# Delta-rule attention with two expert stages: attention's loop written out and its slot reordered

## The reference, cut to what matters

```python
# attention: 4 x 8 heads, 768 steps, head size 48
for t in range(S):
    y[:, :, t] = einsum('bhd,bhde->bhe', q[:, :, t], state)
    v_old = einsum('bhde,bhd->bhe', state, k_n[:, :, t])
    state += beta[t] * einsum('bhd,bhe->bhde', k_n[:, :, t], v[:, :, t] - v_old)
x = y as (3072 tokens, 384)
out = sum_e p_e * (relu(x @ w1[e]) @ w2[e])        # 4 experts, 384 -> 1024 -> 384
out = (sigmoid(out @ w_gate) * (out @ w_val)) @ w_out   # 384 -> 1536 -> 384
```

## Time and profile before

| | us |
|---|---|
| three timed runs | 1962.07, 1930.34, 1958.16 |
| their median | 1958.16 |
| the profiled execution | 1943.01 |
| its span, first to last instruction | 1940.7 |
| attention, from the start to the end of slot 11 and the tail | about 664 |
| slots 1 to 10, ten slots | 517.9 |

### The profile page before, as it was taken

The page is one execution under the profiler, slowest core; times in us unless marked ns, Lnnn a source line. Parts: engine busy times, 40 slices in busy tenths (PEclk is TensorE's granted clock), DMA queues, the critical chain, the costliest instruction groups (busy, mean ns, idle before and its releaser), DMA issues. The chain is left out here.

```text
span 1940.7 us, 42069 instructions
## 1 busy us (share of the span) xinstructions
PE 1838.7 (95%) x18050; PEld 1579.6 (81%) x18050; DVE 662.0 (34%) x1269; ACT 497.8 (26%) x944; POOL 66.4 (3%) x51
## 2 busy tenths in 40 slices
PE   5899989898999799999999999999998999999999
PEld 4677767676677689999999999999997888888888
DVE  6555545454554222222222222222224422222221
ACT  2443334333332121112111121111113322222222
POOL 1000000000000103000300030000000000000000
PEclk9887768787777699999999999999999999999999
DMA  7222222222000321022110301020102100000000
GB/s 154 46 55 48 52 54 54 54 54 54 18 19 19 115 98 66 33 71 91 49 50 32 130 33 66 33 89 33 66 0 73 49 17 17 1 16 16 0 17 17
DMA packets 145512, 95.11 MB, mean 49 GB/s; under 512 B 80944, under 2 KB 125232, under 8 KB 145360
## 3 DMA queue, kind: packets, MB, share of 16 engines
q1 hardware_dynamic: 145360, 92.77, 16.9%
HBM read 78.59 MB, written 14.16 MB: 48 GB/s over the span
## 5 line engine op out<-in xcount | busy, mean ns | idle before, releaser
L947 DVE SCALAR_TENSOR_TENSOR hl<-ebank,hh 128x512 fp32r<-128x512 f32 x192 | 132.9, 692 | 577.0 <-ACT hh L904 577.0
L904 ACT ACTIVATE hh<-ebank 128x512 fp32r<-128x512 f32 x192 | 115.0, 599 | 664.7 <-PE ebank L976 664.7
L974 PE MATMUL ebank<-w2l,hh 128*128 128x384 f32 x768 | 258.6, 337 | 4.1 <-DVE w2l L925 2.3
L976 PE MATMUL ebank<-w2h,hh 128*128 128x384 f32 x768 | 258.6, 337 | 0.0
L975 PE MATMUL ebank<-w2h,hl 128*128 128x384 f32 x768 | 257.8, 336 | 0.0
L974 PE MATMUL ebank<-xl,w1h 128*128 128x512 f32 x576 | 224.7, 390 | 12.2 <-DMA xl<-x_lo 12.2
L976 PE MATMUL ebank<-xh,w1h 128*128 128x512 f32 x576 | 228.0, 396 | 0.0
L975 PE MATMUL ebank<-xh,w1l 128*128 128x512 f32 x576 | 227.6, 395 | 0.0
L605 PE MATMUL bank<-c 128*128 128x256 f16 x576 | 141.7, 318 | 46.5 <-ACT XX L379 22.4
L974 PEld LDWEIGHTS ebank<-w2l,hh 128*128 128x128 f32 x768 | 144.3, 188 | 12.5 <-DVE w2l L925 2.8
L975 PEld LDWEIGHTS ebank<-w2h,hl 128*128 128x128 f32 x768 | 144.2, 188 | 7.0
(11 more groups left out here) (144 smaller groups left out, 2718.4 us busy)
## 6 DMA issues: line engine op xcount, KB each, us to landing
xh<-x_hi SPq DMA_DIRECT2D x24, 768.0 KB, 4.4
xl<-x_lo SPq DMA_DIRECT2D x24, 768.0 KB, 6.0
brep<-in_beta SPq DMA_DIRECT2D x24, 256.0 KB, 5.1
w1raw<-in_moe_w SPq DMA_DIRECT2D x4, 1536.0 KB, 9.6
w2raw<-in_moe_w SPq DMA_DIRECT2D x4, 1536.0 KB, 12.0
k_raw<-in_k SPq DMA_DIRECT2D x12, 384.0 KB, 4.7
v_raw<-in_v SPq DMA_DIRECT2D x12, 384.0 KB, 6.0
q<-in_q SPq DMA_DIRECT2D x12, 384.0 KB, 4.4
```

The costliest lines, as they stand in the source:

```text
L904: nc.scalar.activation(hs[i][0][:, :], bank[i][:, :], ACT.Relu).then_inc(hh_done, 1)
L947: nc.vector.scalar_tensor_tensor(out=hs[i][1][:, :], in0=bank[i][:, :], scalar=0.0, in1=hs[i][0][:, :].bitcast(F32), op0=ALU.max, op1=ALU. ...
L974: mm(dst, stat[0], mov[1], start=first, stop=False)
L976: return mm(dst, stat[0], mov[0], start=False, stop=last)
```

## The change

The loop is gone: all twelve slots are written out, on all engines. In the slot:

- on PE, dense pieces and tile steps are dealt out anew. `u0(0)` stands right behind `first(0)`; `turn(0)` and `turn(1)` move up, to right behind `z1(0)` and `z1(1)`; `s(1)` moves between `m32y(0)` and `m32y(1)`;
- `product_q` is split into its matmuls and, one step later, its mask on DVE (`mask_q`);
- `keep` moves from the slot before to the slot itself;
- the copies of the four quadrants into `XTf` leave `z3` and become a step of their own, `quads`, behind both `m32y`: ACT makes two of the four, DVE the other two;
- `Rf` is made by GpSimd;
- `busy` matmuls: one in place of two in `y1` to `y3`, `z0` to `z3`, `m32y` and `m64y`, none in `y0`. A slot has 28 of them.

```diff
             lev("first", w, p, 0)
+            r("u0", 0)
             lev("first", w, p, 1)
-            r("u0", 0)
+            pre("product_q", w, p, 0)
             lev("y0", w, p, 0)
+            pre("keep", w, p, None)
             n("square")
             r("u0", 1)
             lev("y0", w, p, 1)
-            pre("product_q", w, p, 0)
+            pre("mask_q", w, p, 0)
             lev("z0", w, p, 0)
...
             lev("z1", w, p, 0)
             n("unit", 0)
+            n("turn", 0)
             lev("z1", w, p, 1)
             n("unit", 1)
+            n("turn", 1)
             lev("y2", w, p, 0)
-            n("turn", 0)
+            r("u2", 0)
             lev("y2", w, p, 1)
-            r("u2", 0)
-            n("turn", 1)
+            n("product", 0)
...
             lev("m32y", w, p, 0)
+            r("s", 1)
             lev("m32y", w, p, 1)
-            r("s", 1)
-            n("keep")
+            lev("quads", w, p, 0)
             lev("m32z", w, p, 0)
             rec("z", w, p, 0)
+            lev("quads", w, p, 1)
             lev("m32z", w, p, 1)
             rec("z", w, p, 1)
             lev("m64y", w, p, 0)
             n("turn_q", 0)
             lev("m64y", w, p, 1)
+            lev("m64z", w, p, 0)
             n("turn_q", 1)
-            lev("m64z", w, p, 0)
             lev("m64z", w, p, 1)
...
-            slot(0, 0, lev, rec, pre, has_rec=False)
-            slot(1, 1, lev, rec, pre)
-            slot(2, 0, lev, rec, pre)
-            with eng.Fori(2, NCH) as c:
-                slot(2 * c - 1, 1, lev, rec, pre)
-                slot(2 * c, 0, lev, rec, pre)
-            slot(NW - 1, 1, lev, rec, pre, has_pre=False)
+            for w in range(NW):
+                slot(w, w % 2, lev, rec, pre, has_rec=w > 0, has_pre=w < NW - 1)
...
+                def rec(step, w, p, o):
+                    if step == "z":
+                        pool.wait_ge(r_done, 2 * w + o + 1)
+                        nc.gpsimd.tensor_copy(Rf[o][:, :, :], R[o][:, :, :]).then_inc(rf_done, 1)
...
-                    if step == "z3":
-                        if isinstance(w, int) and w < 2:
+                    if step == "quads":
+                        if w < 2:
                             act.wait_ge(x_zeroed, 1)
                         past(act, u2_rdy, 2 * (w - 1))
                         act.wait_ge(xt_done, 10 * w + 8 + hf + 1)
-                        for b in range(NB):
+                        for b in (2, 3):
...
+                    if step == "quads":
+                        past(dve, u2_rdy, 2 * (w - 1))
+                        for b in range(2):
+                            nc.vector.tensor_copy(XTf[p][quarter(b), half(hf), quarter(b)], XX[hf][quarter(b), 1, :, :])
...
                             pe.wait_ge(x1_done, 2 * w + hf + 1)
-                        busy(ybank[hf])
...
+                        pe.wait_ge(xt_done, 10 * w + 2 * n + hf + 1)
                         busy(xbank[hf])
-                        pe.wait_ge(xt_done, 10 * w + 2 * n + hf + 1)
                         pe.wait_ge(yc_done, 8 * w + 2 * n + hf + 1)
-                        busy(ybank[hf])
```

More of the change, by code:

```diff
@@ L206, in slot @@
             lev("y1", w, p, 1)
+            pre("mask_q", w, p, 1)
             r("au", 1)
@@ L219, in slot @@
             lev("z2", w, p, 1)
-            n("product", 0)
+            r("y", 0)
             lev("y3", w, p, 0)
-            r("y", 0)
+            n("product", 1)
             lev("y3", w, p, 1)
             n("value")
-            n("product", 1)
+            r("y", 1)
             lev("z3", w, p, 0)
-            r("y", 1)
             lev("z3", w, p, 1)
@@ L240, in slot, with run @@
             lev("m64y", w, p, 1)
+            lev("m64z", w, p, 0)
             n("turn_q", 1)
-            lev("m64z", w, p, 0)
             lev("m64z", w, p, 1)
-        def run(eng, lev, rec, pre):
+        def run(lev, rec, pre):
             for step, which in (("square", None), ("norm", None), ("value", None), ("unit", 0), ("unit", 1),
-                                ("turn", 0), ("turn", 1), ("product", 0), ("product", 1), ("keep", None),
+                                ("turn", 0), ("turn", 1), ("product", 0), ("product", 1),
                                 ("turn_q", 0), ("turn_q", 1)):
                 pre(step, 0, 0, which)
-            slot(0, 0, lev, rec, pre, has_rec=False)
-            slot(1, 1, lev, rec, pre)
-            slot(2, 0, lev, rec, pre)
-            with eng.Fori(2, NCH) as c:
-                slot(2 * c - 1, 1, lev, rec, pre)
-                slot(2 * c, 0, lev, rec, pre)
-            slot(NW - 1, 1, lev, rec, pre, has_pre=False)
+            for w in range(NW):
+                slot(w, w % 2, lev, rec, pre, has_rec=w > 0, has_pre=w < NW - 1)
             for step in ("u0", "au", "u2", "y"):
@@ L346, in _ @@
                 reload(0, 1, 0)
[L347 to L357, removed]
+                for w in range(1, NW):
+                    if w + 2 < NW:
+                        reload(w, w // 2 + 1, w % 2)
+                    for o in range(2):
+                        store(w - 1, (w - 1) // 2, (w - 1) % 2, o)
+                for o in range(2):
+                    store(NW - 1, NCH - 1, 1, o)
                 for o in range(2):
@@ L370, in _, with none @@
                 last.then_inc(s_zeroed, 1)
+                def rec(step, w, p, o):
+                    if step == "z":
+                        pool.wait_ge(r_done, 2 * w + o + 1)
+                        nc.gpsimd.tensor_copy(Rf[o][:, :, :], R[o][:, :, :]).then_inc(rf_done, 1)
+                def none(*_):
+                    return
+                run(none, rec, none)
             @block.scalar
@@ L410, in rec @@
                 def rec(step, w, p, o):
-                    if step == "z":
-                        act.wait_ge(r_done, 2 * w + o + 1)
-                        copy(Rf[o][:, :, :], R[o][:, :, :]).then_inc(rf_done, 1)
                     if step == "u0":
@@ L447, in pre @@
                         copy(Ah[p][:, half(which), :], A32[p][:, half(which), :], ASC).then_inc(ah_done, 1)
-                run(act, lev, rec, pre)
+                run(lev, rec, pre)
             @block.vector
@@ L510, in rec @@
                         past(dve, ds_rdy, 2 * (w - 1) + o + 1)
-                        if isinstance(w, int) and w == 0:
+                        if w == 0:
                             dve.wait_ge(s_zeroed, 1)
@@ L577, in pre @@
                                                     ALU.mult).then_inc(ap_done, 1)
-                    if step == "product_q":
+                    if step == "mask_q":
                         dve.wait_ge(qp_rdy, 2 * w + which + 1)
@@ L587, in _ @@
                 last.then_inc(x_zeroed, 1)
-                run(dve, lev, rec, pre)
+                run(lev, rec, pre)
             @block.tensor
@@ L610, in lev @@
                     if step == "first":
-                        if isinstance(w, int) and w == 0 and hf == 0:
+                        if w == 0 and hf == 0:
                             pe.wait_ge(consts_in, 32)
@@ L785, in pre @@
                         product(which, 1).then_inc(qp_rdy, 1)
-                run(pe, lev, rec, pre)
+                run(lev, rec, pre)
 def experts(nc, x_hi, x_lo, w1, w2, probs, acc, w1raw, w2raw, w1_in, ahead):
```

6 lines of the change are left out of this document (2 added, 4 removed).

## The result

The changed kernel takes **2001.86 us** (median of four runs, 1983.86 to 2009.36), the kernel before 1953.59 in the same comparison (four runs, 1930.34 to 1962.07): ratio 1.0274, 95% interval 1.0148 to 1.0401. It is slower; the interval leaves open whether by more or by less than 2%. The forecast was 1914 us, with a range up to 1980.

A forecast was written before the change was run, and what follows sets the result against it. PE was taken to bound the attention slots, by its clock, its waits for ACT and "issue" gaps. 1943.0 - 16.6 - 24 - 36.7 + 13 + 5.5 + 35 - 10 = 1909, plus 5: 1914 us, range 1868 to 1980.

The forecast's parts named there:

- Loop written out, -16.6: In attention, PE's three double "issue" gaps at the branches after slots 4, 6 and 8 go: -16.6 us.
- Busy matmuls, -24: Leaving out 20 of 48 busy matmuls a slot saves 0.10 to 0.11 us each at full clock: -24 us.
- Quadrants behind `Yc`, -36.7: PE's waits for ACT in m32y(1) and m32z(0) go entirely: -36.7 us.
- `z(0)`, +13: PE waits 1.1 to 1.2 us for S(0) from DVE ahead of z(0), in eleven slots: +13 us.
- `m64y(1)`, +5.5: DVE's quads copies delay m64y(1) by between nothing and 1.05 us; half taken: +5.5 us.
- `Rf` on GpSimd, 0: GpSimd's copy is hidden, as u0(0) reads it only some 4 us later: 0 us.
- the rival built on it: GpSimd locks DVE out in quads(1), 0.4 to 1.0 us ahead of m32z(1): 1922 us or so, chance 0.09.
- `turn` moved up, +35: PE waits for ku 1.5 us at turn(0) and 1.9 us at turn(1), in eleven slots: +35 us.
- Clock, -10: Half-clock time in slots 1 to 10 costs 6.9 us a slot against 8.3 before: -14, taken as -10 us.
- I take it back at the end of `y(0)`: The clock lost at the turns returns at the end of y(0), after 11 us at half, costing 4.3 us.
- Until it returns in m64 or in `product_q(0)` that is 8.5 us at half: The wait ahead of z(0) takes the clock in perhaps three slots of four, for 8.5 us, costing 2.6.
- the clock doesn't return: PE stays at 1.2 GHz from the turns to the next slot's product_q: +88 us, 2002 us, chance 0.14.

The follow-up runs named there:

- experiment 1: The kernel before with only its loop written out; 1921.5 us, ratio 0.9859.
- experiment 4: The kernel before with its loop written out and the quadrant copies moved behind Yc, shared by ACT and DVE, nothing else; 1904.7 us, ratio 0.9762.
- experiment 6: The kernel of experiment 4 with 28 busy matmuls a slot in place of 48, placed as in the change; 1916.5 us, ratio 0.9784.
- Experiment 2: The changed kernel with turn, u2, product and y back at their places of before; 1939.4 us, ratio 0.9956.
- 7: The kernel of experiment 4 with only the start of the slot spread as in the change, 48 busy matmuls; 1902.9 us, ratio 0.9747.
- (10): The changed kernel with twelve busy matmuls ahead of each turn's wait for ku, from slot 1 on; 1886.1 us, ratio 0.9614.
- experiment 9: The changed kernel with both unit steps moved earlier, right behind norm, turns left in place; 1878.9 us.
- experiment 11: The kernel of experiment 4 with XTf copied by GpSimd, XTb by ACT, and twelve more busy matmuls a slot; 1850.3 us, ratio 0.9482.
- experiment 3: The changed kernel with its 48 busy matmuls a slot put back; 2012.9 us.
- experiment 12: The changed kernel with both unit steps early, XTf on GpSimd, XTb on ACT and 48 busy matmuls a slot; 1817.6 us, ratio 0.9293.

## Why the prediction was wrong

*Loop written out, -16.6*: right, with a few us more by the clock; alone it gave 23 us by the medians (experiment 1). That written-out slots show no such gap was read too kindly: slot 0 of before has one of 1.9 us.

*Busy matmuls, -24*: the price was right, the gain was not. In the order of experiment 4 they hold the clock, and without twenty of them a slot the kernel is no faster (6).

*Quadrants behind `Yc`, -36.7*: in the change both waits are gone, as forecast.

*`z(0)`, +13*: 12.3 us in eleven waits of 1.1. *`m64y(1)`, +5.5*: none; of the bounds, zero held.

*`Rf` on GpSimd, 0*: right. The copy takes 0.507 us (a row of its group is below), and nobody waits for it. DVE's next pair of casts takes 0.22 us longer beside it, 0.80 instead of 0.58. By the Trainium skill (SBUF — State Buffer, "SBUF: two separate sides") the two share ports under an exclusive lock. The trace agrees: the second cast of the pair starts 0.14 us into the copy and ends 0.14 us behind the copy's end. The 0.2 us are less than the rival built on it had (0.4 to 1.0), and PE has no wait ahead of `m32z(1)`.

*`turn` moved up, +35*: 35.1 us of waits less the 2.5 of before, +33.

*Clock, -10*: **this is the step that failed.** The terms above sum to 1943.0 - 16.6 - 24 - 36.7 + 12.3 + 33 = 1911; the profiled execution took 2003.94, which leaves 93 us for the clock where the forecast had -10. The windows say the same: 438 us at half clock against 207, times 0.4, is +92. The number that went into -10 was built of two parts. "I take it back at the end of `y(0)`" was right to the step (509.8), though it took 17 us from 492.8 and not 11. "Until it returns in m64 or in `product_q(0)` that is 8.5 us at half", in three slots of four, was wrong: it falls behind `z(0)` in each of the ten slots, and stays at half for 27.3 us (13.7 in slot 1), through `m64`, `first`, `product_q(0)`, `z0` and `au(0)` to `au(1)`. The 8.5 came from one place, the return at 223, 9 us into slot 4, and from the end of m64 in slot 8. The trace of before has more than that: with the same order of steps the clock was back 10.2 us after it fell in slots 1, 5, 6 and 8 (in 1, 5 and 6 it fell once more soon after), and 23.9 us after it in slots 2, 3, 9 and 10. A single value for the return could not be read from it. That the return before was helped by its two dummies ahead of each tile step and its dense pieces in a row is argued, not shown.

The rival "the clock doesn't return" gave 2002 and the median is 2002, but its mechanism was half right: it has the clock gone from the turns to the next `product_q`, while in fact it came back at `y(0)` for 10.2 us in each slot and was lost again at `z(0)`. The agreement of the numbers is partly luck. Its chance, 0.14, was too small: I had a sentence in hand that speaks for it, 20 fewer dense matmuls and pieces spread evenly, and let the clock count as a gain of 10 us all the same.

Whether the spreading in the middle of the slot (`product` one tile step earlier, `s(1)` between the `m32y`) has a part of its own in the 27.3 us was not tried alone. Experiment 2 (the change with its turns back) has 333 us at half clock, experiment 6 (28 busy matmuls, quadrants moved, turns in place) has 245. The 88 us between them, 35 us at 0.4 and 34 by the ratios, belong to what else differs: the place of `s(1)`, `Rf`, the order in m64, the start. Part of it is again a wait: `s(0)` waits 1.5 us for `ylo` in each slot of experiment 2 and 1.0 in experiment 6. By 7 the start alone has no effect; the others stay open.

## What to carry to other kernels

Price a wait of TensorE by what it does to the clock, not by its length alone: here, filling waits of 3.1 us a slot without shortening them took 10.8 us off a slot (10), and removing them 13.8 (9). Before a step is moved up, look on the other engine at what makes its input: moved in front of its producer it only waits, and moving the producer too (`unit`) was worth 123 us. And a dummy matmul has no fixed worth: twenty fewer a slot gained nothing (6), twelve more gained 14 to 22 us (11), twenty more beside unfilled waits gained nothing (3). Hold its 0.1 us against the granted clock of the slots, with and without.

## What the runs showed of the hardware that was not expected

*The clock is lost to waits that are short, and a busy PE doesn't bring it back by itself.* In the change it stays at half for 27.1 us in which the profile shows PE busy in 27.10 of 27.10. So it is not idleness alone that keeps it down; what the work must have was not measured by itself. Twelve dummies more in experiment 11 kept it at full in seven slots of ten.

*The same wait does not always take the clock, and the same work does not always bring it back.* In experiment 9 PE waits 1.12 or 1.13 us ahead of `z(0)` in every slot from 2 on. In slots 4, 6 and 8 the clock falls 1.4 to 1.7 us after that wait and is back 13.7 us later; in slots 5, 7 and 9 it doesn't fall.

```profile
332.70:346.40 13.70, 13.70 (x188) 10.64 (x180) 5.64 (x14) 5.68 (x10) 1.01 (x2) 0.50 0.50 105
374.50:414.60 40.10, 38.28 (x999) 31.18 (x1000) 30.64 (x74) 17.56 (x38) 1.01 (x2) 1.00 0.37 75
```

The first window is the stretch at half clock behind the wait of slot 6. The second begins with the end of the wait in slot 7 and goes on to the fall in slot 8. In the change the same PE order from `z(0)` on stays at half for 27.3 us. What decides between the cases is not shown.

*A program can lock into a slow round.* Eight slots of the change take 57.9 to 58.3 us each; experiment 3 runs at 51 us for three slots and at 61.4 from then on. It can also leave such a round: in experiment 2 slots 5 to 7 take 58.0 to 58.3 us, the next three 50.4 to 50.9. A small difference of orders then decides over many slots, and a sum per slot extrapolates badly.

*Code without branches has "issue" waits too.* In experiment 12 PE stops for 2.76 us in slot 8 and starts again 8 us behind the slot's start; the stretch ahead has the DMA engines at 0.86 with 157 GB/s, since SP loads the next k, v and q there. Three of the ten slots have such a wait, of 1.3 to 2.8 us; the clock falls with it each time, and the slot lasts 44.8 to 47.0 us instead of 38.9. The DMA view of this run lists a queue `q8 instruction`. From 349.3 to 358.3 it moves nothing while the loads keep the engines 83% busy; its next packet, of 16 KB, is over by 359.7, and PE starts again at 360.99. That speaks for code that came late behind the loads. It isn't shown: slot 7, with the same loads at 163 GB/s and nothing on that queue from 308.9 to 315.3, has no wait, and no run took the loads away.

*A GpSimd copy slows DVE's casts a little.* The group of GpSimd's copy in the change:

```profile
L368 POOL CAST Rf<-R x24: 502/507/507, 61.0 to 687.2; 128x384 fp32r<-128x384 f32 x24
```

and the cast of 32x256 on DVE that starts beside it takes 0.51 us instead of 0.28, in all twelve slots.
